# Attention scaled on the output bank, unread products in the head, three score banks there and kept weight splits, in a kernel of attention and two feed-forward layers

## The reference

```
attention: q, k, v of shape (2, 8, 768, 64), n_sink = 4, window = 128
  scores = q k^T / 8, kept where key < n_sink or 0 <= query - key < window
  a = exp(scores - rowmax);  a = a / (rowsum + 1e-9);  out = a v
x  = out, reshaped to (1536 tokens, 512)
x  = max(0.01 h, h) @ w_out,  h = x @ w_in        (512 -> 2048 -> 512)
y  = silu(h2) @ w_out2,       h2 = x @ w_in2      (512 -> 2048 -> 512)
```

## Time and profile before

| | |
|---|---|
| median of 3 runs | 679.57 us (679.01 to 680.44) |
| profiled execution, span from first to last instruction | 677.8 us |
| its own device time | not listed apart; the runs lie 1.2 to 2.6 us above the span, their median 1.8 |
| PE busy | 634.3 us, 94% of the span |
| DVE busy | 415.4 us, 61% |
| ACT busy | 362.4 us, 53% |
| POOL busy | 99.3 us, 15% |

### The profile page before, as it was taken

One profiled execution on the slowest core, in us unless ns is written; L12 is line 12 of the kernel. 1 busy time (PEld: TensorE's weight loads), 2 busy tenths in 40 slices (PEclk: granted clock), 3 DMA queues, 4 the chain that ended last, 5 costly groups with the idle time before them and its releaser, 6 DMA issues.

```text
span 677.8 us, 9233 instructions
## 1 busy us (share of the span) xinstructions
PE 634.3 (94%) x3048; PEld 529.2 (78%) x3048; DVE 415.4 (61%) x894; ACT 362.4 (53%) x788; POOL 99.3 (15%) x133
## 2 busy tenths in 40 slices
PE   2566799999999999999999999999999999999997
PEld 2565678888887778888888888888888888888886
DVE  7999977888888887886654545333343333433332
ACT  4667766666667666664544446443344434443342
POOL 5544422222324232200000000000000000000000
PEclk9977799999999999999999999999999999999999
DMA  6343981211121120000222221000010000100001
GB/s 145 110 113 111 297 261 34 47 48 33 48 47 33 48 63 17 1 1 1 93 94 93 94 94 31 1 0 1 1 62 1 0 1 1 58 6 0 1 1 62
DMA packets 12334, 36.50 MB, mean 54 GB/s; under 512 B 2048, under 2 KB 2048, under 8 KB 12288
## 3 DMA queue, kind: packets, MB, share of 16 engines
q1 hardware_dynamic: 12288, 35.92, 18.1%
HBM read 32.77 MB, written 3.15 MB: 53 GB/s over the span
## 4 chain that ended last, share of the span: by engine, by line
PE 62%; DVE 22%; ACT 8%; issue 6%; DMA 1%; ACTq 0%; SPq 0%; DVEq 0%
PE y_ps L808 29%; PE h_ps L781 29%; DVE sm L515 4%; DVE prob L597 4%; DVE pT L524 3%; DVE g_f L559 3%; ACT g L428 2%; ACT g_f L417 2%; DVE g L569 2%; DVE x L537 2%; DVE psT L529 1%; DVE row_inv L590 1%; PE o_ps L748 1%; ACT prob L355 1%; ACT win L400 1%
## 5 line engine op out<-in xcount | busy, mean ns | idle before, releaser
L781 PE MATMUL h_ps<-x,win 128*128 128x512 f32 x1152 | 284.0, 391 | 0.5 <-DVE win L544 0.5
L781 PEld LDWEIGHTS h_ps<-x,win 128*128 128x128 f32 x1152 | 212.8, 188 | 42.6 <-DVE win L544 0.8
L808 PE MATMUL y_ps<-g,wout 128*128 128x512 f32 x576 | 145.7, 393 | 0.0
L808 PE MATMUL y_ps<-wout,g 128*128 128x512 f32 x576 | 138.2, 389 | 0.0
L569 DVE TENSOR_TENSOR g<-g_f,g 128x512 fp32r<-128x512 f32 x96 | 70.9, 739 | 91.7 <-ACT g L421 85.4
L551 DVE TENSOR_TENSOR wout<-w_raw,wout 128x512 fp32r<-128x512 f32 x96 | 72.4, 754 | 86.9 <-ACT wout L408 86.7
L808 PEld LDWEIGHTS y_ps<-wout,g 128*128 128x128 f32 x576 | 108.1, 188 | 22.5
L808 PEld LDWEIGHTS y_ps<-g,wout 128*128 128x128 f32 x576 | 103.9, 188 | 18.6
L408 ACT ACTIVATE wout<-w_raw 128x512 fp32r<-128x512 f32 x96 | 60.2, 627 | 90.9 <-PE y_ps L808 90.9
L355 ACT ACTIVATE prob<-sm,neg_max 128x260 f32<-128x260 f32 x96 | 48.7, 508 | 43.3 <-DVE neg_max L515 42.7
L419 ACT ACTIVATE g_f<-h_ps 128x512 f32<-128x512 f32 x48 | 28.7, 598 | 69.3 <-PE h_ps L781 69.3
(11 more groups left out here) (72 smaller groups left out, 507.2 us busy)
## 6 DMA issues: line engine op xcount, KB each, us to landing
w_raw<-w SPq DMA_DIRECT2D x32, 512.0 KB, 3.5
qk_raw<-qk SPq DMA_DIRECT2D x48, 260.0 KB, 4.2
v_raw<-vt SPq DMA_DIRECT2D x12, 256.0 KB, 2.6
y<-qk_raw SPq DMA_DIRECT2D x12, 256.0 KB, 2.2
vs_raw<-vsink SPq DMA_DIRECT2D x8, 8.0 KB, 3.5
```

The lines of the kernel that those rows point to most:

```text
L781: ins = mm(h_ps[:, :], win[:, F % 2, wp, c * P:(c + 1) * P], x[:, xp, c, i * BLK:(i + 1) * BLK], start=(c == 0 and wp == HI and xp == HI), ...
L808: ins = mm(y_ps[d][:, :], a[:, d * P:(d + 1) * P], r, start=(f == 0 and wp == HI and gp == HI), stop=(f == FT - 1 and wp == LO))
```

## The change

1. **Scaling.** `normalise` goes. `prob` stays unscaled. For each half DVE adds 1e-9 to four row sums and takes their reciprocals, each written 64 times (128 x 256, `invert_sums`); PE turns these in two transposes together with the sinks' (`turn_half`); DVE copies them out (`take_half`, which also splits the sinks, without ACT) and multiplies the output bank by them into `att` (`scale_half`). ACT and POOL split `att` into x.
2. **Unread products.** PE runs 24 matmuls of zeros (bf16, 128x512) at the start and 4 in each of the 19 iterations of the head, into y_ps1, which nobody reads. Scores there use three banks.
3. **Narrow tiles.** The first tile of each sequence uses 128 columns instead of 260, and half the transposes and value matmuls of a pair; tiles 0, 1, 6 and 7 have no sink products (their sinks are in the panel).
4. **Head.** 19 pairs instead of 20. Steps of the body start one iteration earlier, and what x needs still ends in iteration 2e + 4 of half e.
5. **Layer 0.** ACT applies Prelu twice from h_ps; `leaky` and the rounding go.
6. **Weights.** Eight splits stay resident; blocks run through the slices alternately up and down. 64 splits of each weight instead of 96, 64 loads instead of 32, through a ring of four.

```diff
-            return (s_ps, h_ps, y_ps[0], y_ps[1])[n % 4] if n < LEAD * H else s_ps
+            if n < S_THREE:
+                return (s_ps, h_ps, y_ps[0])[n % 3]
+            return s_ps if n >= S_TWO or n % 2 == 0 else y_ps[0]
...
+        def width(T):
+            return P if T % TPB == 0 else PAN
...
+    def has_sinks(T):
+        return T % TPB >= 2
...
+    FS = PAIRS * TB + 3
+    LAST = NPAIR + 4
...
+    turned_in = {2 * e + 3: e for e in range(NHALF)}
+    inverted_in = {2 * e + 2: e for e in range(NHALF)}
+    scaled_in = {2 * e + 4: e for e in range(NHALF)}
...
         @block.gpsimd
+            def low_x(e):
+                pool.wait_ge(x_high, e + 1)
+                nc.gpsimd.tensor_tensor(x[:, 1, rows, cols], att[:, :, :], x[:, 0, rows, cols].bitcast(F32),
+                                        ALU.subtract).then_inc(x_ready, 1)
...
         @block.scalar
+            def high_x(e):
+                act.wait_ge(att_ready, e + 1)
+                nc.scalar.activation(x[:, 0, 2 * half:2 * half + 2, T * P:(T + 1) * P], att[:, :, :],
+                                     ACT.Copy).then_inc(x_high, 1)
...
+            def take_hidden(F):
+                func, slope = (ACT.Prelu, 0.01) if F < N_L0 else (ACT.Silu, 0.0)
+                act.wait_ge(h_done, F + 1)
+                nc.scalar.activation(g_f32[:, F % 2, :], h_ps[:, :], func, alpha=slope)
+                wait(act, y_done, F - 1)
+                nc.scalar.activation(g[:, 0, F % 2, :], h_ps[:, :], func, alpha=slope).then_inc(h_taken, 1)
...
         @block.vector
-            def normalise(u):
...
-                for i in range(2):
-                    a = prob[:, at + i, :]
-                    nc.vector.tensor_scalar(a, a, row_inv[:, u % 2, 1, i:i + 1], None,
-                                            ALU.mult).then_inc(prob_ready, 1)
...
+            def take_half(e):
+                k = job["half", e]
+                dve.wait_ge(t_written, k + 1)
+                bank_ = t_bank(k)
+                if has_sinks(e // 2):
+                    wait(dve, o_done, e)
+                    nc.vector.tensor_copy(psT[:, :], bank_[:, 2 * P:3 * P]).then_inc(sink_step, 1)
+                nc.vector.tensor_copy(scale[:, :, :], bank_[:, 0:2 * P].rearrange("p (c n) -> p c n", c=2)).then_inc(
+                    scale_ready, 1)
...
+            def invert_sums(e):
+                dve.wait_ge(exp_done, 4 * (e + 1))
+                nc.vector.tensor_scalar_add(sum_eps[:, :], row_sum[:, e % 2, :], 1e-9).then_inc(norm_step, 1)
+                dve.wait_ge(norm_step, 2 * e + 1)
+                nc.vector.reciprocal(row_inv[:, :, :],
+                                     sum_eps[:, :].unsqueeze(2).to_broadcast([P, H // 2, D])).then_inc(norm_step, 1)
...
+            def scale_half(e):
+                dve.wait_ge(o_done, e + 1)
+                dve.wait_ge(scale_ready, e + 1)
+                wait(dve, x_ready, e)
+                for lo in (0, D):
+                    src = o_bank(e)[lo:lo + D, :].rearrange("p (c n) -> p c n", c=2)[:, :, 2 * lo:2 * lo + P]
+                    ins = nc.vector.tensor_tensor(att[lo:lo + D, :, :], src, scale[lo:lo + D, :, :], ALU.mult)
...
         @block.tensor
+            def fill(n):
+                for _ in range(n):
+                    mm(y_ps[1][:, :], filler[:, 0:P], filler[:, :].unsqueeze(1).to_broadcast([P, 2, 2 * P]), start=True,
+                       stop=True)
...
+            for a in range(LAST):
+                F = a - FS
+                if a < FS:
+                    if a == 0:
+                        pe.wait_ge(filler_ready, 1)
+                        fill(24)
+                    for n in range(2 * a + 2 if a else 0, min(2 * a + 4, 2 * FS)):
+                        scores(n)
+                    fill(4)
+                    if a in turned_in:
+                        turn_half(turned_in[a])
+                    if a >= 1:
+                        turn_pair(a - 1)
+                    if a >= 2:
+                        weigh_values(a - 2)
+                    if a in turned_in and has_sinks(turned_in[a] // 2):
+                        weigh_sinks(turned_in[a])
+                    continue
+                if a < NPAIR:
+                    scores(2 * a)
+                if a == FS:
+                    hidden(0, 0)
+                    hidden(0, 1)
+                hidden(F + 1, 0)
+                if a in turned_in:
+                    turn_half(turned_in[a])
+                hidden(F + 1, 1)
```

More of the change, by code:

```diff
@@ L332, in _ @@
             low_v(0, 0)
-            for u in range(NPAIR + 1):
+            for u in range(LAST):
                 T, j = divmod(u, PAIRS)
@@ new lines, in _ @@
+            for a in range(LAST):
+                head = a < FS
+                F = a - FS
+                if head:
+                    mask_max(2 * a)
+                    mask_max(2 * a + 1)
+                if a in inverted_in:
+                    invert_sums(inverted_in[a])
+                if 2 <= a <= NPAIR + 1:
+                    low_pair(a - 2)
+                if not head and a < NPAIR:
+                    mask_max(2 * a)
+                if a in turned_in:
+                    take_half(turned_in[a])
+                if a in scaled_in:
+                    scale_half(scaled_in[a])
+                if a == 4:
+                    stack_sink_values()
+                if a == FS:
+                    low_g(0)
+                if not head:
+                    evacuate(F - 1, 1)
+                    if a < NPAIR:
+                        mask_max(2 * a + 1)
+                for s in wout_in.get(F, ()):
+                    low_wout(s)
+                if not head:
@@ L744, in weigh_values @@
                 if u % 2 == 0:
-                    wait(pe, x_ready, freed(o_bank, e))
-                for s in range(2):
+                    wait(pe, att_ready, freed(o_bank, e))
+                only = not has_sinks(T)
+                slots = (0,) if width(T) == P else (0, 1)
+                for s in slots:
                     for vp, pp in PASSES:
@@ L836, in _ @@
-                if 2 <= u <= NPAIR + 1:
-                    weigh_values(u - 2)
-                if T >= LEAD:
-                    project(F, 0)
-                if 1 <= u <= NPAIR and not early:
-                    transposes("pair", u - 1)
-                if u in sinks:
-                    weigh_sinks(sinks[u])
-                if T >= LEAD:
-                    project(F, 1)
-                    F += 1
-                if T == LEAD - 1 and j == PAIRS - 1:
-                    F += 1
-            while F < 2 * NF:
-                hidden(F + 1, 0)
-                hidden(F + 1, 1)
```

665 lines of the change are left out of this document (305 added, 360 removed).

## The result

The changed kernel takes **696.43 us** (median of 4 runs, 695.83 to 698.54), the kernel before beside it 679.44: a ratio of 1.0253, 95% interval 1.0241 to 1.0265. Slower by 17 us, where 662 was forecast and no rival but one ended on that side. The profiled execution has a span of 695.0 us.

What follows compares the result with a forecast made beforehand. DVE was taken to bound the head at 3.88 us a pair, PE the body and rest. 71.1 to step 0 + 585.1 from there + 3.8 stores = 660.0 span; the median lies 1.8 above: 662 us, range 652 to 673.

Steps and rivals of the forecast that it cites:

- DVE idled 4.5 us in the head, and I leave that: Head: DVE's idle time of 77.65 - 73.16 = 4.5 us was taken to stay the same after the change.
- DVE stays last: Head, two pairs: PE 5.5 us, DVE 6.2, POOL near 44 of 61; all close, DVE still the bound.
- The head's sum itself: Head: DVE's instructions in iterations 0 to 18, 45.5 us without reciprocals, plus 10.7 for nine reciprocals, 56.2.
- the 71.1: End of the head: step 0 on PE starts at 71.1 us against 85.95, 14.9 us earlier.
- R: Time of one 256-column reciprocal on DVE, nine in the head: 1.19 us taken, between 0.43 and 2.28.
- The three readings of the two-column row: Reciprocal's extra 8 ns at two columns: start-up cost (0.43 us), 4 ns a column (1.19), all the second column's (2.28).
- the dear end: Highest price weighed for a 256-column reciprocal: 2.28 us, nine of them 20.5 us.
- In the body they hide: Body: dear reciprocals cost no time there, with DVE at 185.06 of 226.60 us before the change.
- the dear rival: Reciprocals of 2.28 us make the head 9.8 us longer and hide in the body: 672 us, chance 0.25.
- Start-up of the body: Iteration 19: half a step of `hidden` 2.7, an iteration with sinks 7.7, step 1's wait for ACT's two passes 1.4.
- the wait before block 1: Body, iteration 34: PE waits some 2.7 us while DVE scales its last half and ACT and POOL follow.
- The slower rival: Head: unread products stand in the way if the clock stays at 0.50, 5.5 us a pair: 704 us, chance 0.05.

Runs made afterwards that it cites:

- experiment 1: Changed kernel without the 100 unread products, three score banks kept: 689.75 us against 696.43.
- experiment 2: Changed kernel without the unread products and with four score banks in the head: 688.48 us.
- experiment 5: Changed kernel with the reciprocal taken of 4 columns and spread by a copy, and placed last in DVE's iteration: 677.69 us.
- the fastest kernel: Kernel of experiment 7 with the head's weight loads and splits spread, and DVE's half of a split one iteration behind ACT's: 668.68 us.
- experiment 8: Kernel before the change with 104 unread products and three score banks in the head added: 678.10 us against 679.44.
- experiment 7: Changed kernel with small late reciprocal, no unread products, four score banks, and the scales' transposes ahead of the scores in the head: 672.28 us.
- experiment 10: Kernel of experiment 7 with the head's weights spread, unread products put where PE waits for the scales, and three score banks: 670.89 us.

## Why the prediction was wrong

- **"DVE idled 4.5 us in the head, and I leave that"; "DVE stays last."** This is the step that failed. From the first mask (10.40 us) to step 0 the forecast had 60.7 us, 56.2 of instructions and 4.5 idle. Measured are 77.45, of which DVE is busy 59.69 and idle 17.76. So of the 16.7 us that step 0 comes late, 13.3 are idle time and 3.5 are work. I had shown that PE, DVE and POOL come to 5.5, 6.2 and near it, and then still added up one engine. With three engines that near, what counts is the order in which each waits.
- **What the runs showed in its place.** With DVE's instructions unchanged, the products behind the scores are 4.8 us of this idle time and the third bank 2.0 (experiments 1 and 2: idle 13.7 and 11.7). The reciprocal's length and place took 11.0 us of busy time out of the head and none of the idle time (experiment 5). Even the fastest kernel idles 9.2 us before step 0. What the 7.2 us that stay between 11.7 and 4.5 hang on is shown by single rows above, not by a run that takes them away.
- **Why 4.5 in the kernel before?** 16.3 us of its DVE time were instructions stretched beyond their shape. While DVE was held up in them, PE had time to get ready. That this hid waits for PE is my reading; experiment 8 fits it, since more work on PE cost nothing there. I had the 0.62 and the 2.00 of the earlier trace rows before me and did not ask what the difference was.
- **The head's sum itself** was sound: with the measured reciprocals it is 45.5 + 15.8 = 61.3, and DVE is busy 59.69. That step 0 came at 73.1 in the last kernel is no confirmation of the 71.1, since a reciprocal with its copy costs 0.47 there, not the 1.19 of the forecast. One slip: the 4.5 was read from 8.30 on and added from 10.40 on; from 10.40 DVE idled 3.7.
- **R.** Middle value 1.19, measured 1.753. On DVE's sum in the head this is 9 x 0.563 = 5.1 us. The three readings of the two-column row were the right ones to weigh, but none was right: 4 columns take 0.178 and 256 take 1.753, so a column costs 1.575 / 252 = 6.25 ns and the start 0.153. The Trainium skill names a repeat count of 8 for the reciprocal ("VectorE: DVE Perf Modes", First, the fixed hardware budget). Read as eight cycles a column that would have been the dear end, 2.28; the trace does not bear that reading out.
- **"In the body they hide"** (DVE's work, in the dear rival, and in the forecast by silence). 9.3 of the 18.3 us from step 0 on are this: DVE is busy 147.43 of 235.42, and yet its reciprocal is on the path, since it stands between PE's last values and the release of their bank. Changing its place or its length removed it alike (9.3 and 9.0).
- **Start-up of the body.** The forecast's terms for iteration 19 are 2.7 + 7.7 + 1.4 = 11.8; measured from step 0 to the next iteration's scores, 15.61 (87.85 to 103.46), 3.8 more. Behind step 0 DVE has two splits that take longer than their 0.69, beside work of POOL (1.26 and 1.80 us at 88.51 and 89.70) ahead of the mask of 92.14, ACT's exponential and then `take_hidden` wait for that mask, PE waits 3.50 at 94.32 and goes on at the lower clock. I had costed step 1's wait as ACT's two passes alone (1.4). Without the products the start-up is 2.1 shorter, with the weights spread 3.3.
- **Right:** the wait before block 1 (2.7, measured 2.64), though not that the clock can fall behind it (+1.7); block 2's wait (0.9, measured 0.93); 5.44 us a step in the rest (measured 5.45); the tail (3.8). Prelu and the second loads at nothing: nothing in the trace of the changed kernel speaks against it, but no run tried either alone, and in experiment 7 a load of q and k was late behind four of weights.
- **The slower rival** had the right culprit and sign and the wrong mechanism. I let the products cost by a low clock; they raised it (0.89 in the head with them, 0.82 without, experiment 1). They cost 6.7 us by standing in front of the scales' transposes. The low clock has a part only in the stalls at 26.42 and 77.00, where they take twice as long. The rival's chance of 0.05 was the chance of one mechanism. That several small waits meet in one loop had no chance of its own.

## What to carry to other kernels

When the bound engine's work comes near the next one's (here 6.2 us against 5.5 for two pairs), stop adding up and lay the two engines' orders beside each other: for each wait, ask what stands between the releasing instruction and the one before it on its own engine. And before counting on what a busy engine will save, compare each of its lines with the shortest time of the same shape; here 16.3 us of 73.16 were more than the shapes need. A long operation that nobody needs yet goes last in its iteration, and an operation whose result is broadcast is done on the narrow operand first (here either alone gave 12 or 13 us, both 18.7). Filling work was free where nothing behind it was waited for (experiments 8 and 10); that place is found in the trace, not by the engine's busy share.

## What the runs showed of the hardware

- **RECIPROCAL on DVE** in fp32: 0.166 us for 2 columns, 0.178 for 4, 1.753 for 256, that is 6.25 ns a column, where a copy with a broadcast operand takes 0.294 for the same 256.
- **A four-column sum on DVE can take 1.30 us.** DVE's row, then POOL's at the same time:

```profile
52.09 1.30 DVE L563 TENSOR_SCALAR sum_eps<-row_sum 128x4 f32<-128x4 f32 x1
```

```profile
52.05 1.30 POOL L328 TENSOR_TENSOR k_hl<-qk_raw,k_hl 128x528 fp32r<-128x528 f32 x1
```

DVE's instruction, 0.159 at best, ends 0.04 us behind the end of POOL's, which had started 0.04 before it. The Trainium skill ("SBUF — State Buffer", Who interferes with whom) says this of DVE in a mode that uses both of its port pairs, which a `tensor_scalar` can enter when its operands meet the conditions: whichever of DVE and GpSimd issues first has the shared pair for its whole instruction, and the other waits. The trace agrees in these two times; that DVE was in such a mode no row shows. The sum's mean was 394 ns in the changed kernel and 215 in experiment 5, where it stands elsewhere in the iteration.
- **The clock.** In the head of the kernel before, 104 unread products raise the mean granted clock from 0.83 to 0.96. In the changed kernel 100 of them do not prevent the lower level behind PE's idle 3.55 us (26.42) and 2.88 us (77.00). The same idle time does not always end in the same way: before block 1 PE waits 2.64 us in the changed kernel and in experiment 1, and the twelve matmuls behind it take 4.42 us in the one and 2.84 in the other.

What stays open: of the 18.3 us from step 0 on, 3.8 are iteration 19, 9.3 the reciprocal and 1.7 the clock behind block 1's wait. The other 3.5 are in amounts too small to assign; 1.2 of them are the four times 0.30 us in which PE waits for its own last values in a half without sinks, which no run took away.
